# Token rows written early, gates in a table of their own, the spread by 32-row pieces and the sort last, in a kernel of attention and two mixtures of experts

## The chip, the cores and the metric

The kernel runs on one core of a Trainium2 chip. The metric is the device time of one execution in microseconds (us); lower is better. The core has five engines with an instruction queue each: TensorE (PE in the profile; PEld are its weight loads), VectorE (DVE), ScalarE (ACT), GpSimd (POOL) and SyncE (SP), which here only issues transfers. Sixteen DMA engines move data between main memory and on-chip memory for the queues of SP, ACT and POOL. TensorE writes into PSUM, eight banks of 128 partitions x 512 f32; only PE, DVE and ACT reach it.

## The reference

```python
def reference(...):
    attn_out = _attn_ref(x, state)                  # x (8, 8, 512, 64), state (8, 8, 32, 64)
    x = attn_out.transpose(0, 2, 1, 3).reshape(4352, 512)
    x = _moe_ref(x, phi, w1, w2)                    # 8 experts x 4 slots, F = 1024
    return _moe2_ref(x, w_gate, w_output_gate, w1, w2)

def _moe_ref(x, phi, w1, w2):                       # soft mixture
    logits = x @ phi                                # (4352, 32)
    slot_input = softmax(logits, over tokens).T @ x
    slot_out = for each expert e: relu(slot_input[e] @ w1[e]) @ w2[e]
    return softmax(logits, over slots) @ slot_out   # c @ slot_out

def _moe2_ref(x, w_gate, w_output_gate, w1, w2):    # each token goes to one expert
    logits = x @ w_gate                             # (4352, 8)
    e_idx = argmax(logits, 1); gate_w = softmax(logits)[e_idx]
    eom = sigmoid(x @ w_output_gate)
    out[t] = gate_w[t] * eom[t, e] * (relu(x[t] @ w1[e]) @ w2[e]),  e = e_idx[t]
```

## The kernel before

The program runs in stages. **Attention** goes over 8 batches and ends at some 100 us. **Soft mixture**: 32 slots pass 8 experts; TensorE multiplies them with the weights of w1 (L724) and of w2 (L742), 2 MB an expert. **Router**: the combine weights c (4352 x 32) give the second mixture's logits (L760); VectorE turns them into the expert, the gate and the place of each token (L1245 to L1364).

The second mixture uses that its input is c @ slot_out, so that x @ w1[e] = c @ (slot_out @ w1[e]). For each expert `hidden_weights(ex)` (L772) multiplies the 32 slots by w1[e]; four blocks of 256 columns lie in the four 32-row groups of a PSUM bank. The result is split into three bf16 parts g1, g2 and g3, whose sum is the f32 value: ScalarE makes g1 (`part_1`, L996), VectorE the rest (`part_rest`, L1236), ScalarE g2 of the rest (`part_2`, L1000), GpSimd g3 (`part_3`, L440). `spread(ex)` on TensorE then copies the parts with picking matmuls into other rows: gA gets g1, g1, g1, g2 in its four groups of 32 rows, gB gets g2, g2, g3, g3. ScalarE copies the four banks into gA and gB (`spread_out`, L1008); for the last two experts VectorE does two of the four (L1373). TensorE's order is hidden product ex, then spread ex - 1, and the sort stands before hidden product 6.

Each token's row in the main-memory table `token_rows` is its c in bf16 pieces (80 words; copies at L423 to L431 on GpSimd) and its gate (word 80, L1276 on VectorE). SyncE's queue writes the table after load 20 of the weights, in 16 transfers (L340, L343), as soon as rows and gates are both there. **Sort**: 34 matmuls (L813) of one-hot matrices put the token numbers in order of expert and tile; VectorE makes the list `sidx` of them (L1358 to L1364).

**Tiles**: tokens of one expert fill tiles of 128 rows, 35 here. GpSimd gathers a tile's rows through the list (L456 copies 128 numbers, L464 is the indirect DMA), four tiles ahead. TensorE turns them (`turn_c`, L846 and L847; the matmuls run two tiles ahead), multiplies by gA and gB (`hidden`, L857 and L858, one tile ahead), ScalarE and VectorE apply relu, and `output` (L869) multiplies by w2[e] in f32. ScalarE scales by the gate (L1046), which it copied out of the gathered row before (L1030), and GpSimd scatters the tile to the output (L456, L474). Filler transposes (`keep_clock`, L517) stand where TensorE waits.

Nothing but each queue's own order and semaphores sets the order. SyncE issues the weight loads u = 0 to 23 (w1 and w2 of the soft mixture, w1 of the second), each as soon as the unit before it in the same memory slot has been used, and then the 8 loads of the second mixture's w2. Load 21 needs `g_psum` 1, that is hidden product 0.

## Time and profile before

| | |
|---|---|
| median of 3 runs | 516.5 us (514.47 to 520.13) |
| profiled execution | 513.55 us, span 511.8 us |
| busy TensorE, its weight loads | 450.1 us (88%), 249.7 us (49%) |
| busy VectorE, ScalarE, GpSimd | 135.8, 143.9, 139.7 us |
| output matmuls L869 | 560 instructions, 249.2 us, mean 598 ns |
| mean granted TensorE clock | 0.957 |
| SP's queue | 77.27 MB, 42.2% of 16 engines' span |

Shares are of the whole span. A group's line gives what it took in all, the mean of one, and the idle time of the engine just before it with what ended it. One f32 matmul is recorded as two instructions. The chain that ended last is followed back from the last instruction, at each step to what released it. PEclk is the granted clock as a share of 2.4 GHz.

### The profile page before, as it was taken

The page shows a single profiled execution, that of the slowest core. Times are in us where ns is not written, and L with a number is a line of the kernel's source. Part 1 is how long each engine was busy: PE and PEld are TensorE (multiplying, and loading weights), DVE is VectorE, ACT ScalarE, POOL GpSimd, SP SyncE. Part 2 cuts the span into 40 slices and gives each one's busy share as a digit, 9 for nine tenths or more (in the row PEclk, how much of TensorE's full clock was granted, in tenths as well). Part 3 has the DMA queues.
Part 4 walks back from the last instruction along what each step waited for, and adds up shares of the span by engine and source line. Part 5 has one row for each costly group of instructions (what it writes and reads, how often), then busy time and mean ns, then how long its engine had stood idle before and what let it go on. Part 6 is the DMA issues. An engine that isn't in the chain of part 4 may idle for free.

```text
span 511.8 us, 10146 instructions
## 1 busy us (share of the span) xinstructions
PE 450.1 (88%) x3556; PEld 249.7 (49%) x3557; DVE 135.8 (27%) x278; ACT 143.9 (28%) x330; POOL 139.7 (27%) x207
## 2 busy tenths in 40 slices
PE   3788986799846967799999999999999999999991
PEld 3467764563304644554545545455454545545440
DVE  1389998820000695210101001010110101101000
ACT  2687864301000363421212212121121212212110
POOL 3154523046000121403323232232323323232110
PEclk9899999899886697999999999999999999999997
DMA  8869635859999979868775010110101011010110
GB/s 251 291 248 338 242 126 214 323 172 363 387 387 408 408 240 405 317 215 279 239 235 184 27 47 24 47 41 30 44 27 47 24 47 43 27 47 21 43 43 2
DMA packets 42691, 88.35 MB, mean 173 GB/s; under 512 B 6143, under 2 KB 15363, under 8 KB 42657
## 3 DMA queue, kind: packets, MB, share of 16 engines
q1 hardware_dynamic: 37616, 77.27, 42.2%
q0 software_dynamic: 3952, 10.33, 6.0%
q8 instruction: 25, 0.41, 0.3%
q10 hardware_dynamic: 1088, 0.26, 0.2%
q14 instruction: 10, 0.07, 0.0%
HBM read 77.61 MB, written 10.59 MB: 172 GB/s over the span
## 4 chain that ended last, share of the span: by engine, by line
PE 75%; DVE 8%; DMA 7%; issue 4%; SPq 2%; ACT 2%; POOL 1%; POOLq 0%; DVEq 0%; ACTq 0%
PE bank L869 48%; DMA arena<-in_moe_w 5%; PE bank L858 3%; PE bank L857 3%; PE bank L724 3%; PE bank L525 2%; PE bank L772 2%; PE bank L742 2%; PE bank L536 2%; PE bank L517 1%; DMA arena<-in_x 1%; DVE rsum L1115 1%; PE bank L553 1%; DVE rmx L1084 1%; SPq L343 1%
## 5 line engine op out<-in xcount | busy, mean ns | idle before, releaser
L869 PE MATMUL bank<-arena,z 128*128 x560 | 249.2, 598 | 0.9 <-DVE z L1379 0.8
L869 PEld LDWEIGHTS bank<-arena,z 128*128 128x128 f32 x560 | 103.6, 190 | 121.9 <-issue 120.0
L1379 DVE TENSOR_SCALAR z<-bank 128x512 f32<-128x512 f32 x35 | 24.2, 692 | 250.7 <-PE bank L858 250.7
L1046 ACT ACTIVATE z<-bank,tile_gate 128x512 f32<-128x512 f32 x35 | 24.1, 687 | 227.7 <-PE bank L869 227.7
L456 POOL COPY rows_to<-sidx 128x1 int32 (+1 forms) x35 | 6.4, 181 | 152.3 <-ACT z L1046 152.3
L464 POOL DMA_INDIRECT z<-token_rows,rows_from x36 | 37.9, 1054 | 29.0 <-POOL rows_from L456 29.0
L474 POOL DMA_INDIRECT out<-z,rows_to x35 | 35.7, 1019 | 29.8 <-POOL rows_to L456 29.8
L857 PE MATMUL bank<-cT,parts 128*128 128x128 bf16 x280 | 36.4, 219 | 0.5 <-issue 0.5
L858 PE MATMUL bank<-cT,parts 128*128 128x128 bf16 x280 | 36.5, 219 | 0.0
L857 PEld LDWEIGHTS bank<-cT,parts 128*128 x280 | 27.4, 98 | 1.2 <-issue 0.9
L858 PEld LDWEIGHTS bank<-cT,parts 128*128 x280 | 27.4, 98 | 1.0 <-issue 0.5
L772 PE MATMUL bank<-arena,soT 128*32 128x256 f32 x256 | 19.6, 462 | 7.8 <-DMA arena<-in_moe_w 7.8
L440 POOL TENSOR_TENSOR z<-z 128x256 bf16<-128x256 f32 x8 | 6.3, 792 | 71.6 <-ACT z L1000 54.8
L742 PE MATMUL bank<-arena,z 128*32 128x512 f32 x112 | 15.2, 679 | 9.8 <-DMA arena<-in_moe_w 9.8
L405 POOL TENSOR_TENSOR parts<-z,rrec 128x512 f32<-128x512 f32 x16 | 16.4, 1048 | 22.1 <-DVE rrec L1117 22.1
L1039 ACT ACTIVATE z<-bank 128x512 f32<-128x512 f32 x35 | 20.9, 597 | 3.7 <-PE bank L858 3.7
L274 POOL COPY z<-arena 128x2048 f32<-128x2048 f32 x6 | 11.4, 1892 | 34.0 <-PE bank L525 19.2
L525 PE MATMUL bank<-ident,z 128*128 128x128 f32 x128 | 17.4, 280 | 3.2 <-DVE z L274 2.6
L915 ACT ACTIVATE arena<-bank 128x512 f32<-128x512 f32 x32 | 17.6, 607 | 8.5 <-PE bank L525 8.5
L525 PEld LDWEIGHTS bank<-ident,z 128*128 128x128 f32 x128 | 14.7, 144 | 5.2 <-issue 2.3
L772 PEld LDWEIGHTS bank<-arena,soT 128*32 128x32 f32 x256 | 8.9, 130 | 16.0 <-DMA arena<-in_moe_w 8.3
L1008 ACT ACTIVATE parts<-bank 128x512 bf16<-128x512 f32 x28 | 14.4, 595 | 2.7 <-PE bank L793 2.7
(226 smaller groups left out, 488.7 us busy)
## 6 DMA issues: line engine op xcount, KB each, us to landing
arena<-in_moe_w SPq DMA_DIRECT2D x31, 2048.0 KB, 11.8
arena<-in_x SPq DMA_DIRECT2D x8, 1024.0 KB, 6.8
parts<-in_moe_w SPq DMA_DIRECT2D x1, 2048.0 KB, 9.2
token_rows<-z SPq DMA_DIRECT2D x8, 162.0 KB, 2.8
z<-token_rows,rows_from POOLq DMA_INDIRECT x36, 2.6
out<-z,rows_to POOLq DMA_INDIRECT x35, 2.9
z<-in_state ACTq DMA_DIRECT2D x4, 64.0 KB, 2.9
z<-in_state SPq DMA_DIRECT2D x4, 64.0 KB, 2.6
```

Source lines behind the costliest of these rows:

```text
L464: e.indirect_dma_start(row[q][:, :], None, table, bass.IndirectOffsetOnAxis(ap=rows_from[:, q:q + 1], axis=0), bounds_check=last_row, oob_ ...
L474: e.indirect_dma_start(out, bass.IndirectOffsetOnAxis(ap=rows_to[:, q % 2:q % 2 + 1], axis=0), ysb[q % 2], None, bounds_check=last_row, oo ...
L525: mm = e.transpose(pX[g % 2][:, P * j:P * j + P], xr[:, j, P * g:P * g + P], ident[:, :])
L742: mm = e.matmul(pR[32 * q:32 * q + 32, :], hTm[:, a:a + NS], w[:, c, :], start=(ex == 0 and c < 4), stop=(ex == NE - 1 and c >= 4))
L772: mm = e.matmul(pG[ex % 2][32 * q:32 * q + 32, 0:256], soT[:, c, 0:NS], w[:, c, 256 * q:256 * q + 256], start=(c == 0), stop=(c == CD - 1))
L857: e.matmul(dst, gA[:, bass.ds(ex * F + P * c, P)], cT[p][:, 0:P], start=True, stop=False)
L858: mm = e.matmul(dst, gB[:, bass.ds(ex * F + P * c, P)], cT[p][:, P:2 * P], start=False, stop=True)
L869: mm = e.matmul(pY[p][:, :], hT[p][:, c, :], arena[:, bass.ds(ex * UNIT + 512 * c, 512)], start=(c == 0), stop=(c == CF - 1))
L915: e.activation(xT[k % 2][:, g, :], pX[g % 2][:, :], ACT.Copy).then_inc(xt_copied, 1)
L1039: e.activation(hT[p][:, 0:4, :], bank[2 * p][:, :].rearrange("p (c t) -> p c t", c=4), ACT.Relu)\
L1046: e.activation(ysb[p], pY[p][:, :], ACT.Copy, scale=tile_gate[:, q:q + 1])\
L1379: e.tensor_scalar(hT[p][:, 4:8, :], bank[2 * p + 1][:, :].rearrange("p (c t) -> p c t", c=4), 0.0, None, ALU.max).then_inc(relu_v, 1)
```

## The change

The token row loses its gate word (`ROWW` 81 to 80). The gates get a table `token_gates` (4352 x 1), written by ScalarE's queue; GpSimd gathers 128 gates a tile in a second indirect DMA, and ScalarE no longer copies gates out of rows. The token rows are written by SyncE's queue after load 11, in three transfers. The spread takes one 32x32 block of the identity for each piece: row group q (256 columns of the hidden product) goes to bank q, 4 column groups x 2 halves, 32 matmuls in all; each bank then holds the gA and the gB half of the same 256 columns. The sort's matmuls stand after the last spread, and VectorE's part of the sort after its copies of the last spreads.

```diff
@@ block.sync
-            for u in range(8, 21):
+            for u in range(8, 12):
                 load_w(u)
-
-            e.wait_ge(row_ready, 2)
-            for b in range(NB):
-                e.dma_start(table[b * (S + NS):b * (S + NS) + S, :].rearrange("(p j) w -> p j w", j=J),
-                            rowbuf[:, J * b:J * b + J, :]).then_inc(table_out, 16)
-                q, f = b % 4, b // 4
-                e.dma_start(table[b * (S + NS) + S:(b + 1) * (S + NS), :],
-                            rowbuf[32 * q:32 * q + 32, NB * J + f, :]).then_inc(table_out, 16)
-            for u in range(21, NU):
+            e.wait_ge(row_ready, 1)
+            by_batch = table.rearrange("(b r) w -> b r w", b=NB)
+            e.dma_start(by_batch[:, 0:S, :].rearrange("b (p j) w -> p b (j w)", j=J),
+                        rowbuf[:, 0:NB * J, :].rearrange("p (b j) w -> p b (j w)", b=NB)).then_inc(table_out, 16)
+            for f in range(2):
+                e.dma_start(by_batch[4 * f:4 * f + 4, S:S + NS, :],
+                            rowbuf[:, NB * J + f, :]).then_inc(table_out, 16)
+            for u in range(12, NU):
                 load_w(u)
@@ block.gpsimd
-            for ex in range(NE - 2):
+            for ex in range(NE):
                 part_3(ex)
...
+            e.memset(tile_gate[:, :], 0.0).then_inc(row_zero, 1)
...
+            def gather_gate(q):
+                e.sem_inc(gate_turns, 1)
+                e.indirect_dma_start(tile_gate[:, q:q + 1], None, gates,
+                                     bass.IndirectOffsetOnAxis(ap=rows_from[:, q:q + 1], axis=0),
+                                     bounds_check=last_row, oob_is_err=False).then_inc(gate_in[q], 16)
...
                 if not first:
-                    e.wait_ge(gate_saved, t - 3)
+                    e.wait_ge(c_psum, t - 3)
+                    e.wait_ge(gate_in[q], 4 * (t - q))
...
                 scatter(t, q, first and t < 2)
+                with live_tile(e, live, t + 4):
+                    if not isinstance(t, int) or t + 4 < ST:
+                        gather_gate(q)
...
             for t in range(4):
-                if t >= 2:
-                    part_3(NE - 4 + t)
                 gather(t, t, first=True)
+            e.wait_ge(gates_out, 16 * 3)
+            for t in range(4):
+                gather_gate(t)
@@ block.tensor, spread(ex)
                 if ex >= 1:
-                    e.wait_ge(ga_ready, 2 * ex)
-                for q in range(4):
-                    at, cols = half(q)
-                    e.matmul(bank[q // 2][0:64, cols], at[:, 32:96], g1, start=True, stop=True)
-                    e.matmul(bank[q // 2][64:P, cols], at[:, 64:P], g1, start=True, stop=False)
-                    mm = e.matmul(bank[q // 2][64:P, cols], at[:, 0:64], g2, start=False, stop=True)
-                mm.then_inc(spread_a, 1)
...
-                    e.matmul(bank[2 + q // 2][0:64, cols], at[:, 32:96], g2, start=True, stop=True)
-                    mm = e.matmul(bank[2 + q // 2][64:P, cols], at[:, 32:96], g3, start=True, stop=True)
+                    e.wait_ge(g_ready_a, out_by_act(ex))
+                if out_by_dve(ex):
+                    e.wait_ge(g_ready_v, out_by_dve(ex))
+                for k, rows in enumerate(((g1, g1, g1, g2), (g2, g2, g3, g3))):
+                    for r in range(4):
+                        for q in range(4):
+                            at = slice(32 * q, 32 * q + 32)
+                            mm = e.matmul(bank[q][32 * r:32 * r + 32, 256 * k:256 * k + 256], identb[at, at],
+                                          rows[r][at, :], start=True, stop=True)
                 mm.then_inc(spread_psum, 1)
...
             for ex in range(2, NE):
-                if ex == NE - 2:
-                    sort_rows()
                 hidden_weights(ex)
                 spread(ex - 1)
             spread(NE - 1)
+            sort_rows()
@@ block.scalar
-                e.wait_ge(spread_a, ex + 1)
-                for k in range(4 if ex < DVE_FROM else 2):
-                    if k == 2:
-                        e.wait_ge(spread_psum, ex + 1)
-                    a = F * ex + 512 * (k % 2)
-                    e.activation((gA if k < 2 else gB)[:, a:a + 512], bank[k][:, :], ACT.Copy)\
-                     .then_inc(ga_ready if k < 2 else gb_ready, 1)
+                e.wait_ge(spread_psum, ex + 1)
+                for q in range(4 if ex < DVE_FROM else 2):
+                    a = F * ex + 256 * q
+                    e.activation(gAB[:, :, a:a + 256], bank[q][:, :].rearrange("p (k n) -> p k n", k=2),
+                                 ACT.Copy).then_inc(g_ready_a, 1)
...
             part_2(1)
+            e.wait_ge(gate_ready, 1)
+            by_batch = gates.rearrange("(b r) w -> b r w", b=NB)
+            e.dma_start(by_batch[:, 0:S, :].rearrange("b (p j) w -> p b (j w)", j=J),
+                        gate[:, 0:NB * J].rearrange("p (b j) -> p b j", b=NB)).then_inc(gates_out, 16)
+            for f in range(2):
+                e.dma_start(by_batch[4 * f:4 * f + 4, S:S + NS, :],
+                            gate[:, NB * J + f:NB * J + f + 1]).then_inc(gates_out, 16)
...
-                if not isinstance(t, int) or t > 3:
-                    e.wait_ge(y_copied, t - 3)
-                e.activation(tile_gate[:, q:q + 1], row[q][:, GATE_W:GATE_W + 1], ACT.Copy).then_inc(gate_saved, 1)
...
+                e.wait_ge(gate_in[q], 4 * (t - q) + 16)
                 e.activation(ysb[p], pY[p][:, :], ACT.Copy, scale=tile_gate[:, q:q + 1])\
@@ block.vector
-            e.wait_ge(row_ready, 1)
-            e.tensor_tensor(rowbuf[:, :, GATE_W], gate[:, :], st1[:, :], ALU.mult).then_inc(row_ready, 1)
+            e.tensor_tensor(gate[:, :], gate[:, :], st1[:, :], ALU.mult).then_inc(gate_ready, 1)
...
+            part_rest(6)
+            part_rest(NE - 1)
+            for ex in range(DVE_FROM, NE):
+                e.wait_ge(spread_psum, ex + 1)
+                for q in (2, 3):
+                    a = F * ex + 256 * q
+                    e.tensor_copy(gAB[:, :, a:a + 256], bank[q][:, :].rearrange("p (k n) -> p k n", k=2))\
+                     .then_inc(g_ready_v, 1)
+
             e.wait_ge(sort_psum, 1)
...
-            part_rest(6)
-            part_rest(NE - 1)
-            for ex in range(DVE_FROM, NE):
-                e.wait_ge(spread_psum, ex + 1)
-                for k in range(2):
-                    a = F * ex + 512 * k
-                    e.tensor_copy(gB[:, a:a + 512], bank[2 + k][:, :]).then_inc(gb_ready, 1)
```

SyncE's queue before, from the loads of the soft mixture's w2 on (`arena` and `parts` are the weight slots; a row gives line, what is written and read, and the shape):

```order
L309 DMA arena<-in_moe_w 128x8x512 [waits w_used] x7
L309 DMA arena<-in_moe_w 128x4x1024 [waits w_used] x5
L340 DMA token_rows<-z 128x324 [waits row_ready]
L343 DMA token_rows<-z 32x81
...
L343 DMA token_rows<-z 32x81
L309 DMA arena<-in_moe_w 128x4x1024 [waits g_psum] x3
L353 DMA arena<-in_moe_w 128x8x512 [waits w_used] x2
```

and with the change:

```order
L315 DMA parts<-in_moe_w 128x8x512 [waits u_psum]
L315 DMA arena<-in_moe_w 128x8x512 [waits w_used] x3
L345 DMA token_rows<-z 128x8x320 [waits row_ready]
L348 DMA token_rows<-z 4x32x80 x2
L315 DMA arena<-in_moe_w 128x8x512 [waits w_used] x4
L315 DMA arena<-in_moe_w 128x4x1024 [waits w_used] x5
L315 DMA arena<-in_moe_w 128x4x1024 [waits g_psum] x3
L358 DMA arena<-in_moe_w 128x8x512 [waits w_used] x2
```

The three writes of the table stand before load 12 and wait for `row_ready` alone; nothing stands between load 20 and load 21 any more.

TensorE before, around the sort (L813), with hidden product 6 (L772) and a spread (L791 to L800) after it:

```order
L799 MATMUL bank<-z,pick 64x256
L800 MATMUL bank<-z,pick 64x256
L813 MATMUL bank<-z 128x82 [waits lane_ready]
L813 MATMUL bank<-z 128x82 x33
L772 MATMUL bank<-arena,soT 32x256 [waits gr_done,w_in5]
L772 MATMUL bank<-arena,soT 32x256 x15
L791 MATMUL bank<-z,pick 64x256 [waits g3_done,ga_ready,g2_done,g1_done]
L792 MATMUL bank<-z,pick 64x256
L793 MATMUL bank<-z,pick 64x256
```

and with the change, from spread 6 (L803) on to the turning of the first tiles (L849):

```order
L803 MATMUL bank<-z,identb 32x256 [waits g3_done,g_ready_a,g2_done,g1_done]
L803 MATMUL bank<-z,identb 32x256 x31
L803 MATMUL bank<-z,identb 32x256 [waits g_ready_a,g3_done,g_ready_v,g2_done,g1_done]
L803 MATMUL bank<-z,identb 32x256 x31
L817 MATMUL bank<-z 128x82 [waits lane_ready]
L817 MATMUL bank<-z 128x82 x33
L836 TENSOR_LOAD texp [waits sidx_ready,texp_ready]
L836 ISA x2
L529 MATMUL bank<-ident 128x128 x16
L849 MATMUL bank<-identb,z 128x128 [waits row_in0,g_ready_v,g_ready_a]
L850 MATMUL bank<-identb,z 128x128
L849 MATMUL bank<-identb,z 128x128 [waits row_in1,c_copied]
```

The sort has moved behind the last spread, and the list `sidx`, the fillers and the first two tiles now follow it.

GpSimd with the change, from the wait for the list to the gathers of the first four tiles:

```order
L448 MEMSET z 128x320 [waits sort_psum,sidx_ready]
L449 MEMSET tile_gate 128x4
L457 COPY rows_from<-sidx 128x1 [waits table_out,row_zero]
L472 DMA z<-token_rows,rows_from 128x80 [waits from_copied]
L457 COPY rows_from<-sidx 128x1
L472 DMA z<-token_rows,rows_from 128x80 [waits from_copied]
L457 COPY rows_from<-sidx 128x1
L472 DMA z<-token_rows,rows_from 128x80 [waits from_copied]
L457 COPY rows_from<-sidx 128x1
L472 DMA z<-token_rows,rows_from 128x80 [waits from_copied]
L462 DMA tile_gate<-token_gates,rows_from 128x1 [waits gates_out]
L462 DMA tile_gate<-token_gates,rows_from 128x1 x3
```

Parts 3 of experts 6 and 7 no longer stand between the row gathers, and four gate gathers follow them.

## Rows read from the trace of the kernel before

**Rows 1.** The page's part 4: what the chain that ended last was made of.

```profile
PE 75%; DVE 8%; DMA 7%; issue 4%; SPq 2%; ACT 2%; POOL 1%; POOLq 0%; DVEq 0%; ACTq 0%
```

**Rows 2.** Windows by stage: busy us by engine, from the first output matmul on.

```profile
core 0: us, PE busy (x) PEld busy (x) DVE busy (x) ACT busy (x) POOL busy (x), PEclk, DMA share, GB/s
221.00:507.00 286.00, 279.93 (x1152) 139.36 (x1152) 22.89 (x34) 53.01 (x132) 80.75 (x132) 1.00 0.23 78
```

**Rows 3.** Timeline of PE, 205 to 222 us: start us, duration us, group.

```profile
205.03 1.93 PE L772 MATMUL bank<-arena,soT 128*32 128x256 f32 x32 [1.00 <-DMA arena<-in_moe_w]
210.31 0.27 PE L791 MATMUL bank<-z,pick 128*64 128x256 bf16 x1 [1.16 <-POOL z L440]
211.74 1.97 PE L517 MATMUL bank<-ident 128*128 128x128 f32 x16
214.39 0.23 PE L846 MATMUL bank<-identb,z 128*128 128x128 bf16 x1 [0.57 <-ACT cT L1033]
217.29 1.26 PE L517 MATMUL bank<-ident 128*128 128x128 f32 x10
221.11 1.12 PE L869 MATMUL bank<-arena,z 128*128 x2 [0.78 <-DVE z L1379]
```

**Rows 4.** Chain that ended last, 120 to 200 us: start us, us, what.

```profile
135.81 19.93 DMA arena<-in_moe_w
184.44 1.81 SPq L343
186.30 7.85 DMA arena<-in_moe_w
194.19 3.64 PE bank L772 x32
```

**Rows 5.** Windows around the table's write; the columns are those of rows 2.

```profile
171.00:174.00 3.00, 3.00 (x36) 1.39 (x32) 2.25 (x7) 0.80 (x2) 0.22 (x1) 0.50 1.02 408
176.65:186.30 9.65, 9.65 (x156) 6.28 (x154) 8.36 (x35) 7.80 (x17) 1.94 (x3) 1.00 0.75 265
186.00:189.00 3.00, 1.39 (x20) 1.12 (x18) 2.88 (x6) 2.39 (x7) 1.42 (x1) 1.00 0.47 101
```

**Rows 6.** Timeline of POOL: the last copy that builds the token rows.

```profile
119.73 2.00 POOL L431 COPY z<-z 128x2176 bf16<-128x2176 bf16 x1
```

**Rows 7.** Issues of the ACT queue (ns min/median/max) and its packets.

```profile
L279 ACTq DMA_DIRECT2D z<-in_state x4: 431/470/479, 0.8 to 2.3; - x4
q10 hardware_dynamic: 1088, 0.26, 0.2%
```

**Rows 8.** Timeline of ACT, PE and DVE, 180 to 213 us.

```profile
182.73 0.38 ACT L996 ACTIVATE z<-bank 128x256 bf16<-128x256 f32 x1
186.03 0.38 ACT L996 ACTIVATE z<-bank 128x256 bf16<-128x256 f32 x1
207.97 0.42 ACT L1000 ACTIVATE z<-z 128x256 bf16<-128x256 f32 x1 [0.56 <-DVE z L1236]
199.25 1.48 PE L813 MATMUL bank<-z 128*128 128x82 bf16 x34
201.46 0.20 DVE L1364 SCALAR_TENSOR_TENSOR sidx<-z 128x41 int32<-128x41 f32 x1
211.85 1.29 DVE L1373 CAST parts<-bank 128x512 bf16<-128x512 f32 x2 [1.37 <-PE bank L800]
```

**Rows 9.** Timeline of PE: products of 32x32 pieces in the attention part.

```profile
106.31 0.85 PE L685 MATMUL bank<-z 32*32 32x64 f32 x64
```

**Rows 10.** Row gathers: the second one, all of them, the one at 215.2.

```profile
205.66 1.02 POOL L464 DMA_INDIRECT z<-token_rows,rows_from  x1 [0.81 <-POOL rows_from L456]
DMA to landing us min/median/max: 2.2/2.6/6.7
z<-token_rows,rows_from POOLq DMA_INDIRECT x1, 3.1
```

**Rows 11.** Window of 1 us in a pause of TensorE; columns of rows 2.

```profile
191.00:192.00 1.00, 0.00 (x0) 0.00 (x0) 1.00 (x1) 0.00 (x0) 0.00 (x0) 0.55 1.02 418
```

45 lines of the change are left out of this document (18 added, 27 removed).

## The prediction

> **What bounds the kernel now.** I read the page's chain first: 75% of what ended last is TensorE [rows 1]. That share hides two stages. From 221.1 us the 35 tiles run, and TensorE works 279.9 of 286 us there [rows 2]; a tile costs some 8 us, nearly all of it f32 output matmuls, and nothing in the change touches them. So the time can move only before the first of these, at 221.11 us [rows 3]; what stands behind it, 290.7 us of span, is carried over. Next the chain of waits from 120 to 200 us, to see which wait ends last there [rows 4]: weight loads hold it from 135.8 to 155.7 us, then comes the router, then SyncE's queue writes the token table until 186.25 us, and only after that is load 21 issued, whose data release TensorE at 194.15. Last the windows from the side of the transfers [rows 5]: 408 GB/s before the table, 265 while it is issued, 101 just after. Full is a DMA share of 1.03; 9.65 us at 0.75 and 3 us at 0.47 lose about 4.0 us. That hole is what the change can close.
>
> **Step 1, table written early.** The token rows are ready when GpSimd's last copy ends at 121.7 us [rows 6]. Loads 9 to 11 are then still in the queue, so SyncE's short wait leaves no gap. But the table now stands ahead of loads 12 to 15, on which TensorE waits. Its price: in the window of 9.65 us 2.56 MB moved in 7.0 us of full share [rows 5]; 1.377 MB were table, the rest at 408 GB/s takes 2.9 us, so the table takes 4.1 us (336 GB/s). Load 15 lands at 155.7 + 4.1 = 159.8, and the whole router moves by +4.1. Lower bound 3.4 us, the table at 408 GB/s.
>
> **Step 2, no hole.** Load 21 needs only that the first hidden product is done, some 176 us, while loads 17 to 20 are still in the queue. So eight loads of 2.097 MB follow load 15 at 5.14 us each (408 GB/s), 41.1 us: load 23 lands at 200.9, against 205.0 (start of the product of expert 7, [rows 3]).
>
> **Step 3, gate table.** ScalarE issues three DMAs at about 181 us, 0.47 us each by its issues at the start [rows 7]: 1.4 us before spread 0 is copied out. ScalarE's cycle is 3.3 us an expert [rows 8], the loads' 5.14, so by expert 7 it has over 2 us to spare: nothing on the path. The transfers are 1,280 packets of 16 or 4 bytes. The nearest small packets, those of ScalarE's queue, are 1,088 in 0.2% of 16 x 511.8 us [rows 7], 15 ns each: 1.2 us on 16 engines, and I take 1.0. The bounds are nothing and the 51 ns of a table packet (4.1 x 16 / 1,280), 4.1 us. Load 23 is then at 201.9, a gain of 3.1.
>
> **Step 4, the spreads.** Twenty 64-column matmuls (1.4 us, 210.31 to 211.74, [rows 3]) become 32 pieces of 32x32. The kernel has such pieces, 32 products (64 instructions) in 0.85 us, but with 64 columns [rows 9]; with 256 I put a spread between 0.8 and the old 1.4 and take 1.3. Two stand in the last stretch, so the lower bound gives 1.0 back. ScalarE and VectorE copy the same 512 elements a bank.
>
> **Step 5, the end of the spreads.** Now part 3 of experts 6 and 7 stands behind GpSimd's gathers, and spread 7 waits for it until 210.31 [rows 3]; this goes. Product 7 ends at 201.9 + 1.93 = 203.8, parts 1 and 2 end 1.4 later (206.96 to 208.39 now, [rows 3, 8]), the copies of expert 6 some 1.2 after that (VectorE's pair takes 1.29, [rows 8]), and spread 7 takes 1.3: it ends at 207.9, against 211.8. So far the change has won 3.9 us.
>
> **Step 6, sort and gathers, now last.** The sort's 34 matmuls ran at 199.25 and the gathers under the last spreads, at no cost. Now: 1.5 us for the sort, 0.9 from its end to the list (200.73 to 201.66, [rows 8]), ready at 210.3; VectorE's copies of expert 7 lie beside the sort. From the list to the start of the second gather are 4.0 us (201.66 to 205.66, [rows 8, 10]), 4.1 with the memset of the gates: 214.4. TensorE is in order and turns tile 1 before the hidden product of tile 0, so the second gather counts. A gather lands after 2.2 to 6.7 us, median 2.6 [rows 10]; the one at 215.2, in the gap between two loads as here, took 3.1, and here the next load is nearer, so 3.7: 218.1. From turning tile 1 to the first output matmul are 6.7 us (214.39 to 221.11, [rows 3]), hence 224.8.
>
> **Step 7, clock.** TensorE now idles from about 212 to 218 but for two transposes. After its work stopped near 187.4 (1.39 us of it in the window from 186, [rows 5]) the granted clock was down to 0.55 in 191 to 192 [rows 11], then 0.50 (1.2 GHz of 2.4), and the next product took 3.64 us for 1.93 [rows 3, 4]. I let only the ten filler transposes pay, 0.12 us each at full clock [rows 3]: +1.1. First output matmul at 225.9, **+4.8 us**.
>
> **Costed at nothing.** The 35 gate gathers: GpSimd's step has two indirect DMAs, each with its copy and wait some 2.1 us (0.81 and 1.02 of it in [rows 10]), of a tile's 8.0; a third of 1.0 to 2.1 still fits. If it didn't, ScalarE's scaling would wait, then TensorE. The removed gate copies lie in ScalarE's idle time. The tail keeps its scatter.
>
> **Sum.** Spread 7's end moves from 211.8 to 207.9 (-3.9); from there to the first output matmul it was 9.3 us and is 1.5 + 0.9 + 4.1 + 3.7 + 6.7 + 1.1 = 18.0 (+8.7); together +4.8. The profiled execution took 513.55 us (span 511.8), which gives 518.3; the median of the runs, 516.5, is 3 us above it, so **521.3**. A measurement of this kernel tells about 1%, 5.2 us, from no change: the forecast is just inside that. Its own range: table 3.4 (-0.7), gates 0 (-1.0), spreads (-1.0), gather 2.2 (-1.5), no clock loss (-1.1) make -0.5 in all, 516; gates 4.1 (+3.1) and gather 6.7 (+3.0) make +10.9, 527.4.
>
> **Rivals.**
>
> A, *the small writes crowd few engines* (slower). The order shows the state rows and the gates as transfers whose outer dimension is 4 (4x32x80, 4x32x1), where there were eight of 32 rows. If such a transfer runs on four of the 16 DMA engines, these carry 64 table packets each, 3.3 us at 51 ns, less the 0.8 they had, and 64 gate packets at 15 ns, 1.0; a load lands with its slowest engine, so every later landing moves by 3.4: 524.7, and 528 if a gate packet costs 51 ns. It decides as soon as the four are as busy as the rest, and the share is 1.0 throughout; no view shows single engines.
> By the Trainium skill (DMA: Bandwidth & Descriptors, section "Why a DMA increments its semaphore by 16 and not by 1") a DMA of the hardware queues uses the largest number of engines up to 16 that divides the slowest dimension of both sides, which would be four here; by that rule A's 524.7 holds, without it 521.3.
>
> B, *the win is kept* (no change). If the gathers land in 2.2 us and the clock does not fall, 516 to 518.7. Against it: weight loads run on beside these gathers, and TensorE idles longer than the 4 us after which its clock had fallen.
>
> C, *the 32x32 pieces run one after the other*. At 0.107 us for 256 columns a spread takes 3.4 us, the cycle with the four copies 5.5, above the loads', and the last spread ends some 15 us later: 536. Against it: pieces start 27 ns apart [rows 9].
>
> D, *faster by over 1%*: the first output matmul would have to start before 216, well below the lower bound. Only if the table costs loads 12 to 15 nothing (writes beside reads), together with B: 220.6 - 3.4 = 217.2, 512.6. Against it: in the table's window the reads did not keep 408 GB/s.
>
> **Chances.** Forecast 0.45, A 0.27, B 0.17, C 0.04, D 0.07. Slower by over 1% are A, C and a good quarter of the forecast's own range: 0.43. Faster is 0.05 (most of D). Same is 0.52. The range goes from B's end with a part of D, 514.5, to A's end, 528.
>
> **What would show it.** Right: no window under 350 GB/s between 125 and 200 us; the table's DMAs issued at 122 us; the wait for load 15 ending near 160, for load 23 near 202; the last spread ending near 208; then TensorE idle for some 6 us with the second gather as what it waits for; output from 226. Wrong: load 15 near 163 and load 23 past 204 (A); spreads over 2 us (C); load 15 still at 156 (D); the tile loop longer than 290.7 us.

## The result and the profile after

| | before | with the change |
|---|---|---|
| median | 516.15 us (514.47 to 520.13, 4 runs) | 534.24 us (529.63 to 535.08, 4 runs) |
| ratio | | 1.0345, interval 1.0308 to 1.0383 |
| profiled execution | 513.55 us, span 511.8 | 533.59 us, span 531.8 |
| mean granted clock | 0.957 | 0.929 |

The change made the kernel 18 us slower; 521.3 had been forecast, with a range of 514.5 to 528. The result lies above the range. The two profiled spans differ by 20.0 us, and that sum closes over four marks: the end of the last spread, the start of the first output matmul, its length, and what follows the tile loop.

The timeline of PE with the change (start us, duration us, group, in brackets the idle time before and what ended it), against [rows 3]:

```profile
187.49 0.66 PE L803 MATMUL bank<-z,identb 32*32 32x256 bf16 x32 [6.50 <-ACT parts L1009]
188.07 3.64 PE L784 MATMUL bank<-arena,soT 128*32 128x256 f32 x32
...
208.55 0.66 PE L803 MATMUL bank<-z,identb 32*32 32x256 bf16 x32 [7.42 <-ACT parts L1009]
...
215.44 0.44 PE L803 MATMUL bank<-z,identb 32*32 32x256 bf16 x32 [2.07 <-ACT parts L1009]
215.81 1.48 PE L817 MATMUL bank<-z 128*128 128x82 bf16 x34
...
224.30 0.27 PE L849 MATMUL bank<-identb,z 128*128 128x128 bf16 x1 [2.69 <-DMA z<-token_rows,rows_from]
...
228.04 2.34 PE L529 MATMUL bank<-ident 128*128 128x128 f32 x10
231.54 0.22 PE L849 MATMUL bank<-identb,z 128*128 128x128 bf16 x1 [1.16 <-DMA z<-token_rows,rows_from]
...
235.31 9.98 PE L872 MATMUL bank<-arena,z 128*128 x16 [0.70 <-ACT z L1044]
```

The last spread ends at 215.88 us (211.74 before): +4.1. From there to the first output matmul are 19.4 us (9.4 before): +10.1. That group takes 9.98 us where the same 16 take 7.13 at full clock: +2.85. This last part is of this execution and not of the change: in experiments 7 and 14, whose kernels are the same up to this group but for GpSimd's order in the tiles, it takes 7.13 us. Tile 0 is turned after a wait of 2.69 us for its gather, and the next turning that waits for a gather is that of tile 2, at 231.54. Both spreads with a long wait (6.50 and 7.42) wait for ScalarE's copies, and the reason of each is on another engine.

ScalarE's timeline with the change shows the first (ACTq rows are issues of transfers):

```profile
179.97 0.41 ACTq L1022 DMA_DIRECT2D token_gates<-gate  x1
180.42 4.81 ACTq L1025 DMA_DIRECT2D token_gates<-gate  x2
185.28 2.07 ACT L1009 ACTIVATE parts<-bank 128x512 bf16<-128x512 f32 x4 [6.13 <-issue]
...
206.04 0.42 ACT L1003 ACTIVATE z<-z 128x256 bf16<-128x256 f32 x1 [7.33 <-DVE z L1242]
```

The three gate writes hold ScalarE for 5.3 us (0.41, 1.12 and 3.66, the issues one by one), and the copies of spread 0, which began at 177.11 before, begin at 185.28. The last row, part 2 of expert 5, points to VectorE. Its timeline with the change:

```profile
195.62 0.42 DVE L1242 TENSOR_TENSOR z<-bank,z 128x256 f32<-128x256 f32 x1
195.96 1.60 DVE L1343 TENSOR_TENSOR z<-tau,dtile 128x1394 bf16<-128x1394 f32 x1
197.59 5.04 DVE L1346 TENSOR_TENSOR z<-lane,dlane 128x4352 bf16<-128x4352 bf16 x1
202.56 3.12 DVE L1349 TENSOR_TENSOR z<-z,idf 128x1394 bf16<-128x1394 bf16 x2
205.60 0.41 DVE L1242 TENSOR_TENSOR z<-bank,z 128x256 f32<-128x256 f32 x1
```

and the same work before:

```profile
186.90 1.60 DVE L1338 TENSOR_TENSOR z<-tau,dtile 128x1394 bf16<-128x1394 f32 x1
188.54 5.04 DVE L1341 TENSOR_TENSOR z<-lane,dlane 128x4352 bf16<-128x4352 bf16 x1
193.50 3.12 DVE L1344 TENSOR_TENSOR z<-z,idf 128x1394 bf16<-128x1394 bf16 x2
198.38 0.42 DVE L1236 TENSOR_TENSOR z<-bank,z 128x256 f32<-128x256 f32 x1 [1.76 <-ACT z L996]
```

These 9.7 us build the one-hot matrices for the sort; the rest of expert 5 stands behind them in VectorE's queue. Before, they lay from 186.90 to 196.6: 7.3 us of them in the hole in which everybody waited for load 21 (until 194.15, [rows 4]), the other 2.4 beside product 5, which ran at the slow clock (3.64 us). The rest of expert 5 came behind them after an idle time of 1.76 us, so they delayed nothing. Now the rest follows at once (no bracket at 205.60), and it is the rest that is late: ScalarE's part 1 of the same expert was done at 198.7.

The part of the chain of waits with the change that answers to [rows 4] says the same in short (start us, us, what):

```profile
181.57 3.66 ACTq L1025
...
202.56 3.12 DVE z L1349 x2
...
224.27 7.13 DMA z<-token_rows,rows_from
235.31 9.98 PE bank L872 x16
```

No load of the second mixture's w1 is in it any more: the hole is closed, as the windows show (columns of [rows 2]), against [rows 5]:

```profile
174.00:186.00 12.00, 6.99 (x116) 3.43 (x108) 8.24 (x27) 2.60 (x8) 1.34 (x2) 0.78 1.03 408
186.00:195.00 9.00, 7.17 (x128) 2.92 (x128) 4.99 (x20) 6.64 (x16) 1.46 (x2) 0.59 1.05 409
...
198.00:201.00 3.00, 2.42 (x64) 1.25 (x64) 3.00 (x1) 0.71 (x2) 0.09 (x1) 1.00 0.70 170
```

What the transfers won, nobody used. The 170 GB/s at 198 to 201 are not for want of work: load 23 had been issued at 181.05 and the first two loads of the second mixture's w2 by 197.40, as SyncE's timeline shows:

```profile
181.46 15.94 SPq L358 DMA_DIRECT2D arena<-in_moe_w  x2
```

Beside them ran the packets of ScalarE's gate writes, from 183.6 to 204.3 us. By the landing events of the traces, load 23 and the first load of w2 land 5.1 and 5.4 us after the load before them in experiment 12, where the gate writes come later; here it is 6.8 and 7.5. These 4 us were not on the path, since product 7 came only at 209.14, but the gate writes were not free for the loads. TensorE's granted clock was 0.59 in the middle window, behind its idle time of 6.50 us.

The end: behind GpSimd's last scatter come 10.66 us (span 531.8), before 7.75 (span 511.8), counted from the end of the scatter's row:

```profile
520.16 0.98 POOL L482 DMA_INDIRECT out<-z,rows_to  x1 [0.82 <-POOL rows_to L457]
```

So 14.2 us up to the first output matmul, 2.85 in it, 2.9 at the end: 20.0. The tile loop between has a mean of some 8.0 us a tile, as before.

### The profile page after: what moved, and what is told of

Read it like the earlier page. It is cut to its first block, busy times and chain, and to the rows that moved or that the text cites. A ratio compares the mean times of both kernels' runs of the same rounds, so it can differ in the third digit from the quotient of the medians.

```text
span 531.8 us, 10382 instructions
## 1 busy us (share of the span) xinstructions
PE 451.6 (85%) x3652; PEld 246.6 (46%) x3653; DVE 136.1 (26%) x278; ACT 141.7 (27%) x295; POOL 175.7 (33%) x239
## 4 chain that ended last, share of the span: by engine, by line
PE 73%; DVE 10%; DMA 6%; issue 4%; ACT 3%; ACTq 1%; POOL 1%; SPq 1%; POOLq 0%; DVEq 0%
PE bank L872 47%; DMA arena<-in_moe_w 4%; PE bank L861 3%; PE bank L860 3%; PE bank L736 3%; PE bank L537 3%; PE bank L784 2%; PE bank L754 2%; PE bank L548 1%; DMA z<-token_rows,rows_from 1%; DVE rsum L1121 1%; PE bank L565 1%; DVE rmx L1090 1%; ACT parts L1009 1%; ACTq L1025 1%
## 5 line engine op out<-in xcount | busy, mean ns | idle before, releaser
L872 PE MATMUL bank<-arena,z 128*128 x560 | 252.0, 604 | 0.8 <-ACT z L1044 0.7
L872 PEld LDWEIGHTS bank<-arena,z 128*128 128x128 f32 x560 | 104.7, 192 | 123.8 <-issue 121.8
L462 POOL DMA_INDIRECT tile_gate<-token_gates,rows_from x36 | 37.5, 1040 | 11.0 <-issue 11.0
L754 PE MATMUL bank<-arena,z 128*32 128x512 f32 x112 | 18.0, 789 | 12.7 <-DMA arena<-in_moe_w 12.7
L272 POOL COPY z<-arena 128x2048 f32<-128x2048 f32 x6 | 11.4, 1893 | 36.8 <-PE bank L537 20.8
L405 POOL TENSOR_TENSOR parts<-z,rrec 128x512 f32<-128x512 f32 x16 | 16.5, 1050 | 20.8 <-DVE rrec L1123 20.8
L537 PE MATMUL bank<-ident,z 128*128 128x128 f32 x128 | 19.9, 309 | 2.2 <-DVE z L272 1.4
L784 PE MATMUL bank<-arena,soT 128*32 128x256 f32 x256 | 21.3, 494 | 0.0
L803 PE MATMUL bank<-z,identb 32*32 32x256 bf16 x256 | 4.6, 338 | 17.6 <-ACT parts L1009 17.6
L537 PEld LDWEIGHTS bank<-ident,z 128*128 128x128 f32 x128 | 16.9, 160 | 4.6 <-issue 1.8
```

Source lines behind the costliest of these rows:

```text
L462: e.indirect_dma_start(tile_gate[:, q:q + 1], None, gates, bass.IndirectOffsetOnAxis(ap=rows_from[:, q:q + 1], axis=0), bounds_check=last_ ...
L537: mm = e.transpose(pX[g % 2][:, P * j:P * j + P], xr[:, j, P * g:P * g + P], ident[:, :])
L754: mm = e.matmul(pR[32 * q:32 * q + 32, :], hTm[:, a:a + NS], w[:, c, :], start=(ex == 0 and c < 4), stop=(ex == NE - 1 and c >= 4))
L784: mm = e.matmul(pG[ex % 2][32 * q:32 * q + 32, 0:256], soT[:, c, 0:NS], w[:, c, 256 * q:256 * q + 256], start=(c == 0), stop=(c == CD - 1))
L872: mm = e.matmul(pY[p][:, :], hT[p][:, c, :], arena[:, bass.ds(ex * UNIT + 512 * c, 512)], start=(c == 0), stop=(c == CF - 1))
```

## The experiments

"Last spread" is the time at which it ends, "output" the start of the first output matmul, both of the profiled execution; before they are 211.74 and 221.11, with the change 215.88 and 235.31. Line numbers shift by some lines from kernel to kernel.

**1. Gates by SyncE** (`gates_by_sync`). The three gate writes leave ScalarE for SyncE, behind load 23.

```diff
@@ block.sync
             for u in range(12, NU):
                 load_w(u)
+            e.wait_ge(gate_ready, 1)
+            by_batch = gates.rearrange("(b r) w -> b r w", b=NB)
...
@@ block.scalar
-            e.wait_ge(gate_ready, 1)
-            by_batch = gates.rearrange("(b r) w -> b r w", b=NB)
...
```

> The changed kernel with the three gate writes issued by SyncE's queue after load 23 instead of by ScalarE. Theory 1 (ScalarE stands still while it issues them, 5.3 us from 179.97 to 185.23, and VectorE and TensorE wait behind it): the copies of spread 0 start near 181.5 instead of 185.3, TensorE's pause of 6.5 us and the half clock after it go, the last spread ends 4 to 5 us earlier, total 4 to 5 us less, some 529.5. Rival (the small writes crowd four DMA engines and the loads are what waits): moving the issue changes nothing, 0 to 1 us. Rival (VectorE's one-hot work sets the end of the spreads whatever ScalarE does): under 2 us.

Measured: 525.42 us (4 runs; ratio 1.0214, 1.0142 to 1.0286). Last spread 211.45, output 230.59. TensorE's timeline:

```profile
182.01 0.44 PE L810 MATMUL bank<-z,identb 32*32 32x256 bf16 x32 [0.48 <-ACT parts L1016]
204.41 0.66 PE L810 MATMUL bank<-z,identb 32*32 32x256 bf16 x32 [6.88 <-ACT parts L1016]
230.59 7.13 PE L879 MATMUL bank<-arena,z 128*128 x16 [0.76 <-DVE z L1386]
```

The wait of 6.50 us before spread 1 is 0.48, and the one behind VectorE's block stays (6.88). The medians are 8.8 us apart, twice the 4 to 5 expected. The stalled issue explains 4.4 to 4.7 of them, by which the last spread and the output come earlier; 2.85 more are the first group at full clock, which experiments 7 and 14 have with the stall in place too, and so are not shown to be the issue's.

**2. Sort where it was** (`sort_kept`). The sort back before product 6, its list before the rests of experts 6 and 7, the gathers between parts 3.

```diff
@@ block.tensor
             for ex in range(2, NE):
+                if ex == NE - 2:
+                    sort_rows()
...
-            sort_rows()
```

> The changed kernel with the sort before hidden product 6 as it was before, VectorE's list before its last rests, and the row gathers between the last parts 3. Theory (the sort at the end lays sort, list and gathers bare, and TensorE's clock falls in that wait): the 10.1 us between the last spread and the first output matmul and the 2.9 us of slow first output come back, 13 us less, some 521; tiles start within 10 us of the last spread. Rival (only the sort's 1.5 us and the list's 0.9 are on the path, the gathers wait for busy DMA engines anyway): 2 to 4 us less, 531.

Measured: 526.42 us (ratio 1.0205, 1.0140 to 1.0271), less good than expected. The output starts at 232.10 and takes 7.13 us; but the last spread ends only at 220.59, since TensorE now waits for VectorE's block before the sort (its timeline):

```profile
207.85 2.50 PE L819 MATMUL bank<-z 128*128 128x82 bf16 x34 [6.46 <-DVE z L1352]
219.93 0.66 PE L805 MATMUL bank<-z,identb 32*32 32x256 bf16 x32 [2.18 <-POOL z L440]
```

From the spread's end to the output it is 11.5 us instead of 19.4. The place of the sort costs 8 us, and VectorE's block would cost whatever the place.

**3. Sort last in the kernel before** (`before_sort_last`). The one move, the other way round, with the diff of experiment 2 reversed.

> The kernel before with the sort alone moved last (TensorE, VectorE's list, GpSimd's parts 3 ahead of the gathers). Theory: last spread up to 1 us earlier, then sort, list, three gathers and a cold clock: 10 to 13 us slower than before, 526 to 529. Rival: 2 to 4 us slower, 519.

Measured: 525.03 us (ratio 1.0182, 1.0127 to 1.0237). The last spread is at 212.94, the output at 233.09, 20.2 us behind it. The theory, then, if just below its 526. Here the second gather decides, as step 6 had it, but tile 1 is turned 7.2 us after its start and not 3.7. GpSimd starts it:

```profile
219.28 1.03 POOL L464 DMA_INDIRECT z<-token_rows,rows_from  x1 [0.82 <-POOL rows_from L456]
```

and TensorE turns tile 1 at

```profile
226.50 0.27 PE L843 MATMUL bank<-identb,z 128*128 128x128 bf16 x1 [6.28 <-DMA z<-token_rows,rows_from]
```

**4. More fillers** (`fillers`). Fifty filler transposes before tile 0, 28 instead of 10 behind the first hidden product.

> The changed kernel with more filler transposes: 50 more ahead of turning tile 0, and 28 instead of 10 after the first hidden product, where TensorE waits for the gathers anyway. Theory (the clock fell to 1.2 GHz in that wait): first output 7.1 us instead of 9.98, fillers hide in the wait: 3 to 4 us less, 530.5. Rival (the fillers hold TensorE longer than the gathers do): 0 to 3 us more.

Measured: 533.14 us (ratio 1.0333, 1.0275 to 1.0391). The output group takes 7.13 us, but starts at 238.57. From the last spread's end (217.75 in this execution) to it are 20.8 us for 19.4. Of the 2.85 us that the clock gave, the length of the fillers took 1.4. The time is 1.1 us under the change's and not the 3 to 4 expected.

**5. The one-hot block spread out** (`gates_sync_onehot_late`). On experiment 1; VectorE's lane matrix in three parts behind the rests of experts 5, 6 and 7, the tile products last.

```diff
+            part_rest(5)
+            lane_part(0, 12)
...
-            part_rest(5)
...
             part_rest(6)
+            lane_part(12, 24)
             part_rest(NE - 1)
+            lane_part(24, NT)
...
```

> The changed kernel with the gates written by SyncE after load 23, and VectorE's 9.7 us of one-hot work behind part_rest(5): the lane one-hot in three parts between and behind the last rests, the tile products last. Theory (VectorE's in-order queue holds back the rest of expert 5, which had a hole of the loads as cover before): with gates by sync alone the spread of expert 5 waited 6.88 us for ScalarE's part and the last spread ended at 211.5; here that wait is under 2 us and the last spread ends 4 to 7 us earlier, near 206. But the sort's inputs are then ready only some 8 us after the last rest, so the sort starts at 211 to 213, no earlier than before: time 524 to 527, about the 525.4 of gates by sync alone. Rival (the copies or the loads set the last spreads, not VectorE's queue): the last spread stays at 210 to 211 and the time rises by 1 to 3 us.

Measured: 530.38 us (ratio 1.0305, 1.0279 to 1.0332), worse than experiment 1. Of the theory, the wait before spread 5 is gone, but the last spread ends at 213.32 and not near 206: it had overlooked that VectorE also copies half of spread 6. TensorE's timeline:

```profile
201.78 3.64 PE L791 MATMUL bank<-arena,soT 128*32 128x256 f32 x32 [4.15 <-DMA arena<-in_moe_w]
205.35 0.65 PE L810 MATMUL bank<-z,identb 32*32 32x256 bf16 x32
212.66 0.66 PE L810 MATMUL bank<-z,identb 32*32 32x256 bf16 x32 [6.66 <-DVE parts L1375]
```

The products of experts 6 and 7 now wait for their loads, as I had forecast for the whole change: product 7 starts at 201.78. The prediction's 201.9 held 1.0 us for the gate writes ahead of load 23, which stand behind it here, so that 200.9 is the figure to compare. But the block of work had only been pushed on, before the copies of spread 6.

**6. Both** (`sort_kept_gates_sync`). Experiments 1 and 2 together.

> The changed kernel with the gates written by SyncE after load 23 and the sort put back before hidden product 6, its list and the row gathers between the parts. What stays of the change: the early table, the 32-row spread, the gate table. Theory (ScalarE's stalled issue and the sort's new place cost 8 to 9 us each and are independent): about 516 to 519, no different from the kernel before. Rival (VectorE's one-hot block now holds the sort, so that part_rest(6) and the last spreads are late whatever the place of the sort): 522 to 526, with the last spread at 215 or later.

Measured: 523.02 us (ratio 1.0158, 1.0128 to 1.0188): the rival. The sort waits 6.56 us for VectorE and runs at 200.55 at the slow clock, the last spread ends at 214.22, the output starts at 227.73. Two repairs that take 8.8 and 7.8 us off alone take off 11.2 together: they are not independent, both end at VectorE's queue.

**7. One branch in GpSimd's step** (`one_if`). The scatter first, then one branch with the row gather and the gate gather.

```diff
             def step(t, q, first=False):
-                with live_tile(e, live, t + 4):
-                    if not isinstance(t, int) or t + 4 < ST:
-                        gather(t + 4, q)
                 scatter(t, q, first and t < 2)
                 with live_tile(e, live, t + 4):
                     if not isinstance(t, int) or t + 4 < ST:
+                        gather(t + 4, q)
                         gather_gate(q)
```

> The changed kernel with GpSimd's step in another order: scatter first, then one branch that holds the row gather and the gate gather of the tile four ahead, where there are two branches around the scatter. Theory (the 2.95 us that the end of the program gained come from the second branch of each step, which GpSimd still has to go through for the tiles behind the last): 1.5 to 3 us off between the last scatter and the end, 531 to 533. Rival (they come from something else, the code size or the tail of the scatter): the same 534.

Measured: 572.97 us (ratio 1.1146, 1.1105 to 1.1186). Every other tile now takes 9.8 to 10.0 us instead of 8.1; the reason is open. Behind the last scatter there are 10.7 us as before: the second branch is not the cause.

**8. The small gate writes first** (`gates_state_first`).

```diff
+            for f in range(2):
+                e.dma_start(by_batch[4 * f:4 * f + 4, S:S + NS, :],
...
             e.dma_start(by_batch[:, 0:S, :].rearrange("b (p j) w -> p b (j w)", j=J),
...
-            for f in range(2):
-                e.dma_start(by_batch[4 * f:4 * f + 4, S:S + NS, :],
...
```

> The changed kernel with ScalarE's three gate writes in another order: the two small ones (4x32x1) first, the large one (128x8x8) last. Theory a (an issue waits for what the issues before it left in the queue, so that position decides, 0.41, 1.12, 3.66 us): the last, now the large one, takes over 3 us. Theory b (the form decides): the two small ones take 1.1 and 3.7 us at the first places too, and the large one 0.4. Time as the changed kernel's, 534, unless the sum of the three falls from 5.2 us.

Measured: 528.72 us (2 runs; ratio 1.0267, 1.0232 to 1.0301), over 5 us off for a swap of two statements. ScalarE's timeline:

```profile
182.53 1.68 ACTq L1023 DMA_DIRECT2D token_gates<-gate  x2
184.25 0.49 ACTq L1025 DMA_DIRECT2D token_gates<-gate  x1
```

2.2 us instead of 5.2. Neither theory holds as I wrote it. The first small write takes 1.12 us in both orders, with nothing ahead of it here and the large one ahead in the change. What the order changes is the second small one, 0.53 us here and 3.66 there: on this queue an issue stood for over 3 us only with the large write of 1,024 packets ahead. SyncE's issues stand too when much is ahead: 5.41 us for the two small writes behind the table's large one, 15.94 for two weight loads behind others. What in the queue sets the limit is not shown.

In the profiled execution the last spread ends 2.3 us earlier than with the change and the output starts 1.5 earlier (233.81); the first group at full clock (7.13 us) makes up the rest of the time. More was not won, since the gate writes now ran beside loads 21 and 22:

```profile
190.00:195.00 5.00, 3.34 (x108) 1.51 (x100) 3.53 (x11) 3.08 (x8) 0.76 (x1) 1.00 0.96 230
195.00:200.00 5.00, 2.65 (x64) 1.25 (x64) 4.97 (x2) 2.68 (x6) 1.46 (x1) 1.00 0.98 275
```

The engines are as busy as ever and move 230 and 275 GB/s for 408. Loads 21 and 22 land 7.6 and 8.1 us after the one before, where 5.14 is usual, and product 6 waits 4.76 us for its load, until 203.47. So small writes did hold up the weight loads, as rival A had it, though at another place.

**9. Three unused semaphores in the kernel before** (`before_3_semaphores`).

```diff
+        spare = [sem(f"spare{q}") for q in range(3)]
```

> The kernel before with three more semaphores that nothing uses: the change has three more than it (nine new ones, six gone). The end of the program behind the last scatter is 7.75 us in both kernels without gate gathers and 10.7 us in all five with them, also where GpSimd's step has only one branch. Theory (each semaphore costs about 1 us when the program ends): 10.5 to 10.9 us behind the last scatter, and 2.9 us on the time. Rival (it hangs on the gate gathers themselves, or on GpSimd's longer code): 7.75 us and no difference.

Measured: 515.29 us (ratio 1.0008, 0.9977 to 1.0038), 7.79 us behind the last scatter. The three semaphores cost nothing at the end.

**10. The 32-row spread alone** (`before_spread32`), the diff of the change for `spread` and its copies, on the kernel before.

> The kernel before with the 32-row spread alone (thirty-two 32x32 matmuls of 256 columns for twenty of 64 rows, a bank per row group, one wait for both halves); table, gates and sort as before. Theory (a spread now takes 0.45 to 0.66 us for 1.43, two of them stand behind the last product, but ScalarE can't begin to copy before the whole spread is done): 514.5 to 516, that is 0 to 1 us faster than before, the last spread ends near 211. Rival (the later start of the copies costs more than the shorter spread gives): 517 to 519.

Measured: 518.05 us (10 runs; ratio 1.0040, 1.0014 to 1.0065): the rival, if barely, and within what counts as no change here. A spread takes 0.44 us at full clock (0.65 to 0.92 at the slow one). In the profiled execution load 23 was 3.4 us later than before and product 7, at 208.46, ran at the slow clock (3.60 us). Load 15, ahead of every spread, was already 1.8 of these 3.4 us later; whether the others are the spread's doing is not shown.

**11. Holding the third load of w2 back** (`gates_sync_hold_v2`), on experiment 1.

```diff
+                if ex == 2:
+                    for q in range(4):
+                        e.wait_ge(row_in[q], 16)
```

> The kernel of gates by sync, but SyncE issues the third load of the second mixture's w2 only when the first four row gathers have landed. Theory (the gathers land 4 to 7 us after their start because their 128 short packets share the engines with the weight loads): the third and fourth land in 2.2 to 3.5 us, tile 2 is turned some 3 us earlier, first output matmul near 227 for 230.6, time 522 to 523 for 525.4. Rival (they are slow for another reason, GpSimd's own queue): landings of 4 to 7 us and the time as with gates by sync.

Measured: 524.74 us (2 runs; ratio 1.0176, 1.0131 to 1.0220), output at 229.79 for 230.59: within the scatter of experiment 1. The third tile is turned at 228.11 without waiting for a transfer, behind the fillers at the slow clock. So taking the weight loads away from the gathers is worth under 1 us there.

**12. `best`**, a version from experiments 1, 2 and 5: sort before product 7 with 20 fillers ahead of it, one-hot work between the rests, the list before rest 7, the gate writes behind the second load of w2.

```diff
@@ block.vector
+            lane_part(0, 12)
             part_rest(5)
+            lane_part(12, 24)
+            id_part(0)
+            lane_part(24, NT)
+            part_rest(6)
+            id_part(1)
...
             part_rest(NE - 1)
@@ block.tensor
+                if ex == NE - 1:
+                    keep_clock(20, pL)
+                    sort_rows()
                 hidden_weights(ex)
```

> A version made from what the runs showed: early table and 32-row spread as in the change; gates written by SyncE behind the second load of the second mixture's w2; VectorE's lane one-hot in three parts and the two tile products between the rests of experts 5 and 6; the sort before hidden product 7, with 20 fillers before it, in the wait for load 23; the list before rest 7; part 3 of expert 7 behind the first gather. Theory: sort at 200.5 to 202, list near 204.5, last spread 208 to 210, third tile turned by 217, first output matmul 217.5 to 220 (221.1 before), the end 2.9 us longer as in all kernels with gate gathers: 513 to 517. Rival (VectorE's queue is still too full, every rest one load late): last spread 212 or later, 519 to 523.

Measured: 523.02 us (ratio 1.0141, 1.0090 to 1.0192). Up to the gathers it nearly came out: sort at 204.19 (200.5 to 202 expected), last spread at 211.06 (208 to 210), first gather started at 208.38. But tile 0 is turned at 218.42 only. The transfers of the 9.5 us from 211.5 on (queue, packets, MB, share of 16 engines):

```profile
q0 software_dynamic: 113, 0.14, 51.2%
q1 hardware_dynamic: 409, 0.16, 27.4%
```

The output, expected at 217.5 to 220, starts at 227.07. 113 packets of the row gathers took half of all engine time, 0.69 us each (51.2% of 16 x 9.5 us), beside the gate writes on SyncE's queue, to which the 392 packets under 512 bytes in this stretch belong. In the kernel before, the gathers' 111 packets from 200 to 215 us took 2.9% of 16 engines, 0.06 each:

```profile
q0 software_dynamic: 111, 0.15, 2.9%
```

**13. `best2`**: the gate writes from there to ScalarE before part 2 of expert 6, small ones first.

> The kernel called best, with the gate writes moved from SyncE (behind the second load of the second mixture's w2) to ScalarE before part 2 of expert 6, where it waits 2.8 us for VectorE, the two small ones first. Theory (in best the 1,280 small packets of the gate writes, 50 to 90 ns each on otherwise idle engines, stood ahead of the row gathers, which took 7 to 9 us to land and set the first tiles): gathers land in 3 to 5 us, the third tile is turned by 220, the first output matmul starts 221 to 223 for 227.1, time 517 to 519. Rival (the gathers are slow for another reason, or ScalarE's issue stalls again): 521 to 525.

Measured: 517.67 us (10 runs; ratio 1.0047, 1.0023 to 1.0071). Tiles 0, 1 and 2 are turned at 213.44, 215.29 and 220.38, the output starts at 222.09. TensorE's timeline:

```profile
202.56 1.48 PE L819 MATMUL bank<-z 128*128 128x82 bf16 x34 [1.65 <-DVE z L1357]
208.91 0.44 PE L805 MATMUL bank<-z,identb 32*32 32x256 bf16 x32 [2.63 <-POOL z L440]
213.44 0.26 PE L853 MATMUL bank<-identb,z 128*128 128x128 bf16 x1 [0.39 <-DMA z<-token_rows,rows_from]
222.09 7.13 PE L876 MATMUL bank<-arena,z 128*128 x16 [0.28 <-issue]
```

That is what the theory had, 16.6 us faster than the change, and 0.5% slower than the kernel before, within the 1% that counts as no change. Its gathers' packets took 0.07 us each. The gate writes on SyncE's queue had cost 5 us. The 1.0 us by which the output is late and the 2.9 us of the end remain.

**14. Gate gathers for the first four tiles only** (`gates_first_four`), on the change.

> The changed kernel with gate gathers for the first four tiles only; the 31 others use the gates that stand there (this leaves part of the computation out: the later tiles are scaled by wrong gates). Theory (the gate gathers in the loop, as transfers or as code that GpSimd has to pass, make the end longer): 7.7 to 7.9 us behind the last scatter for 10.7, time 531 for 534; the tile loop itself stays at 8.0 us a tile. Rival (it is the gate table and its first gathers, or ScalarE's code): 10.7 us and 534.

The kernel leaves the later gates out: 31 tiles are scaled by the gates of the first four. Measured: 528.38 us (2 runs; ratio 1.0240, 1.0198 to 1.0283). Behind the last scatter are 8.06 us. With gate gathers in the loop it is 10.6 to 10.8 in all twelve kernels that have them, without them 7.75 to 8.06 in the five others. So they make the end longer by some 2.6 to 2.9 us. The time fell by 5.9, since the first output group took 7.13 us here. Whether it is the transfers or the code that GpSimd passes on its way out stays open.

**15. `best3`**: `best2` with 16, 26 and 10 fillers in three waits.

> The kernel called best2 with more filler transposes where TensorE waits: 16 before the last spread (it waits 2.6 us for GpSimd's part 3), 26 instead of 16 behind it, 10 between the turnings of tiles 0 and 1. Theory (the slow clock of 212 to 221 us costs the first hidden product, the ten fillers and the third turning some 2.5 us): the clock stays at 1.0 up to the first output matmul, which starts at 219.5 to 220.5 for 222.1; time 514.5 to 516 for 517.7, no longer slower than the kernel before. Rival (the wait for the third gather or the length of the fillers takes its place): 517 to 518.5.

Measured: 519.90 us (10 runs; ratio 1.0069, 1.0040 to 1.0098), worse than both theory and rival. The clock is 1.00 in every window from 206 to 227 us, and from the last spread's end to the output it is as long as in `best2`, 12.7 us. In this stretch the slow clock is not what is paid for.

## Why the prediction was wrong

**Right.** The table's write early cost the router 3.6 us (load 15 landed at 159.3; +4.1 forecast, step 1), and the hole went (step 2). Load 23 landed at 202.3 by the trace's landing events, 201.9 forecast; where no other engine stood in the way (experiment 5), product 7 started at 201.78, with the gate writes behind its load (200.9 by steps 1 and 2). A spread by 32-row pieces takes 0.44 us at full clock, below even the lower bound of 0.8 (step 4); pieces do not run one after the other, and case C fell. From list to second gather 4.0 us (step 6: 4.1). Two sums of the recorded text are off by little: step 5's terms add up to 207.7 and not 207.9, and the table of step 1 is 1.410 MB by its shapes, not 1.377 (0.1 us).

**Case A** is half right. The landings in the trace bear out the rule of the Trainium skill that I had weighed there (DMA: Bandwidth & Descriptors, "Why a DMA increments its semaphore by 16 and not by 1"): the table's large write has 16 and each of its two small ones 4, where all 16 writes of the kernel before have 16 each. At load 15 it was worth no microsecond: A wanted 163. But the gate writes, 1.0 us in step 3 (0 to 4.1), held up load 23 and the first load of w2 by 4.0 us together, and loads 21 and 22 by 5.4 in experiment 8. So there was a window under 350 GB/s before 200 us (265 from 195 on), which the prediction had excluded. In the change this lay off the path.

**Step 3 failed first.** "ScalarE issues three DMAs at about 181 us, 0.47 us each": "nothing on the path". The price came from four transfers of 272 packets each at the program's start [rows 7]; here the third issue, behind 1,152 packets, took 3.66 us. ScalarE stood for 5.3 us (1.4 forecast), TensorE idled 6.50 us, its clock fell to 0.50, and with it product 3 took 3.64 us for 1.93. The spare time of 2 us by expert 7 was too short to absorb that. Experiment 1 takes 4.4 to 4.7 us off the front by it (8.8 between the medians), experiment 8 only 1.5 to 2.3 (5.5).

**Step 5 failed with it, and for a larger reason.** It puts the last spread at 207.9 by following product 7 and the parts, and never looked at what else is in VectorE's queue. The one-hot block of 9.7 us had been free in the kernel before because it lay in the hole, and the change closes that hole. It was not in the sum at all. Product 7 was to end at 203.8 and ends at 212.78, though its load is there at 202.3. The block shows at three places: before part 2 of expert 5 (waits of 6.4 to 7.6 us before spread 5, in the change and experiments 1, 4, 7, 11 and 14), before the sort (6.5 and 6.6, experiments 2 and 6), before the copies of spread 6 (6.7, experiment 5). With the block in pieces and a wait of TensorE before the sort of 1.65 us, experiment 13 has the last spread at 209.35. Instead of -3.9 us the last spread's end moved by +4.1.

**Step 6: mechanism right, the wrong gather.** The second gather landed 2.5 us after its start (3.7 forecast), and TensorE turned tile 1 at 225.15. But from there to the output it was 10.2 us, not 6.7 and 1.1, since the third gather, started at 224.27, took 7.13 us to land. The 3.7 was taken from the gather at 215.2; the first four of the kernel before, with the loads at full rate beside them, had taken 5.3 to 5.8 us (median 5.6). With step 7 the sort's new place was to cost 8.7 us, and it cost 10.1. In the kernel before the same move alone costs 12 us up to the first output (experiment 3).

**Step 7: no fault of the sum.** 1.1 us were put down for ten fillers, and they took 1.1 longer (2.34 for 1.26). The first output group paid 2.85 more in this execution, where two kernels with the same front did not (experiments 7 and 14): as far as the runs show, that is chance, and no term of the sum. Fillers won nothing in experiments 4 and 15.

**"The tail keeps its scatter"**, costed at nothing, was wrong by 2.9 us: with the gate gathers in the loop the program ends later (experiment 14).

Against the sum: last spread 8.0 us too late (steps 3 and 5; 4.4 of them the gate issues by experiment 1), the way from there to the output 1.4 too short, the first group 2.85, the end 2.9. Together 15.2; the profiled execution was forecast at 518.3 and took 533.59. The rivals A, B and D all lay on the side of the transfers; none lay on the queues of ScalarE and VectorE, where 8 of the 15 us were lost.

## What to carry to other kernels

When a change closes a hole, list what every engine does in that hole: each piece of work in it was free and will now stand ahead of something, in order, on its own queue. Price the issue of a transfer on a computing engine by what stands ahead of it in that queue, and keep transfers of many tiny packets away from loads and gathers that somebody waits for: here they cost weight loads up to 5.4 us and, on SyncE's queue, the first gathers 5. Two repairs that end at the same queue do not add up. And compare a slow clock at one place over several kernels before it is put down to the change.

## What the hardware showed that was not expected

- Of three issues on ScalarE's queue, a write of 1,024 packets of 16 bytes and then two of 128 packets of 4 bytes took 0.41, 1.12 and 3.66 us. With the two small ones ahead it was 1.12, 0.53 and 0.49; in `best2` 1.11, 0.53 and 0.50.
- The gate writes, 1,304 packets on ScalarE's queue, took little engine time by the view (0.4% of 16 engines for 0.2% in the whole program), but the weight loads beside them ran at 230 to 275 GB/s for 408 with the engines at a share of 0.96 to 0.98 (experiment 8). On SyncE's queue behind the weights, in experiment 1 from 199.5 to 207 us, 688 packets, 638 of them under 512 bytes, filled 46.5% of 7.5 us with next to nothing else under way, 81 ns each:

```profile
q1 hardware_dynamic: 688, 0.12, 46.5%
```

- Row gathers beside the gate writes on SyncE's queue took 0.69 us a packet instead of 0.06 (experiment 12).
- A row gather of 128 x 320 bytes landed 2.1 to 7.1 us after its issue (median 2.5) with the change, the ones over 3 us all before 270 us, while weight loads were on the queue. The Trainium skill (DMA: Bandwidth & Descriptors, "Anatomy of one DMA — SWDGE (gpsimd) path") gives a transfer from GpSimd a fixed cost of about 2 us and adds the bytes. The fastest agree with it and the median is 0.4 us above; the ones for which TensorE waits do not agree.
- Thirty-two 32x32 by 256-column bf16 matmuls in four row and four column groups took 0.44 us: 14 ns each.
